# Retention into two feed-forward layers: stacked output matmuls for two pairs, small zero matmuls first, and a tile moved into pair 3

## What is computed

```python
def _attn_ref(q, k, v):
    scores = 1.0 / np.sqrt(D_) * np.matmul(q, k.transpose(0, 1, 3, 2))
    gamma = 1.0 - 2.0 ** (-5.0 - np.arange(H))
    rel = pos[:, None] - pos[None, :]
    Dmat = np.where(rel >= 0, gamma[:, None, None] ** rel[None, :, :], 0.0)
    return np.matmul(scores * Dmat[None], v)
...
for e in range(E):
    out += p[:, e:e + 1] * (np.maximum(x @ w1[e], 0.0) @ w2[e])
...
h = x @ w_in
return (h * np.tanh(log1p(exp(h)))) @ w_out
```

## Time and profile before

| what | value |
|---|---|
| median of three runs | 619.76 us |
| the profiled execution's own time | 620.43 us |
| its span (first to last instruction) | 618.7 us |
| TensorE busy | 606.0 us, 98% |
| VectorE, ScalarE, GpSimd busy | 262.9, 234.8, 278.3 us |
| matmul records | 4016 |
| granted TensorE clock, mean | 0.994 |

### The profile page before, as it was taken

One profiled execution on the slowest core, in us unless ns is written; L12 is line 12 of the kernel. 1 busy time (PEld: TensorE's weight loads), 2 busy tenths in 40 slices (PEclk: granted clock), 3 DMA queues, 4 the chain that ended last, 5 costly groups with the idle time before them and its releaser, 6 DMA issues.

```text
span 618.7 us, 9829 instructions
## 1 busy us (share of the span) xinstructions
PE 606.0 (98%) x4016; PEld 546.6 (88%) x4016; DVE 262.9 (42%) x361; ACT 234.8 (38%) x434; POOL 278.3 (45%) x230
## 2 busy tenths in 40 slices
PE   7799999999999999999999999999999999999997
PEld 4688999999899999999999999989989999989996
DVE  2468654424254424154534154535545432324334
ACT  2466333322233322223432223435455454334431
POOL 3558645534435545335553435532446543443300
PEclk9799999999999999999999999999999999999999
DMA  8963312322102332012332102321211232201002
GB/s 339 334 218 103 87 41 65 119 84 68 35 35 68 104 103 68 35 35 68 103 88 66 52 34 69 103 68 46 58 34 58 67 101 83 68 1 52 1 1 102
DMA packets 24923, 50.47 MB, mean 82 GB/s; under 512 B 2864, under 2 KB 2992, under 8 KB 24880
## 3 DMA queue, kind: packets, MB, share of 16 engines
q1 hardware_dynamic: 24736, 49.84, 25.5%
q10 hardware_dynamic: 144, 0.02, 0.0%
HBM read 47.49 MB, written 2.36 MB: 81 GB/s over the span
## 4 chain that ended last, share of the span: by engine, by line
PE 97%; issue 1%; DVE 1%; DMA 1%; ACT 0%
PE bank L494 31%; PE bank L496 31%; PE bank L495 31%; PE bank L442 2%; PE bank L470 1%; DMA loaded<-in_first 1%; PE bank L474 1%; PE bank L612 1%; PE bank L447 0%; PE bank L619 0%; DVE acc_sb L889 0%; DVE acc_sb L893 0%; ACT st L686 0%; DVE h_lo L850 0%; ACT h_hi L717 0%
## 5 line engine op out<-in xcount | busy, mean ns | idle before, releaser
L395 POOL TENSOR_TENSOR w_lo<-w_raw,w_hi 128x512 fp32r<-128x512 f32 x96 | 133.9, 1409 | 148.4 <-ACT w_hi L368 144.9
L494 PE MATMUL bank<-w_hi,h_hi 128*128 128x512 f32 x432 | 168.7, 390 | 0.0
L496 PE MATMUL bank<-w_hi,h_lo 128*128 128x512 f32 x432 | 168.4, 390 | 0.0
L495 PE MATMUL bank<-w_lo,h_hi 128*128 128x512 f32 x432 | 168.3, 390 | 0.0
L876 DVE TENSOR_TENSOR h_act<-part,bank 128x384 f32<-128x384 f32 x96 | 52.9, 551 | 170.4 <-PE bank L496 169.9
L390 POOL TENSOR_TENSOR ws<-ws_f,ws 128x1024 fp32r<-128x1024 f32 x24 | 58.4, 2432 | 144.7 <-ACT ws L364 144.7
L496 PEld LDWEIGHTS bank<-w_hi,h_lo 128*128 128x128 f32 x432 | 81.1, 188 | 16.9
L495 PEld LDWEIGHTS bank<-w_lo,h_hi 128*128 128x128 f32 x432 | 81.1, 188 | 12.3
L494 PEld LDWEIGHTS bank<-w_hi,h_hi 128*128 128x128 f32 x432 | 81.0, 188 | 12.1
L722 ACT ACTIVATE part<-bank 128x384 f32<-128x384 f32 x72 | 35.4, 491 | 138.9 <-PE bank L496 138.9
L843 DVE SCALAR_TENSOR_TENSOR h_lo<-h_act,h_hi 128x384 fp32r<-128x384 f32 x64 | 73.4, 1156 | 20.9 <-ACT h_hi L712 20.3
(11 more groups left out here) (88 smaller groups left out, 863.8 us busy)
## 6 DMA issues: line engine op xcount, KB each, us to landing
w_raw<-in_weights SPq DMA_DIRECT2D x144, 256.0 KB, 2.8
loaded<-in_toks SPq DMA_DIRECT2D x9, 512.0 KB, 6.4
loaded<-in_feats SPq DMA_DIRECT2D x8, 512.0 KB, 5.9
out<-acc_sb SPq DMA_DIRECT2D x6, 256.0 KB, 2.0
out<-acc_sb SPq DMA_DIRECT2D x1, 768.0 KB, 3.5
loaded<-in_first SPq DMA_DIRECT2D x1, 726.0 KB, 4.4
ident<-in_ident SPq DMA_DIRECT2D x1, 64.0 KB, 6.0
p_nat<-in_probs ACTq DMA_DIRECT2D x1, 18.0 KB, 6.4
```

Of the source, the lines that this page charges most:

```text
L395: pool.tensor_tensor(w_lo[layer][:, x], w_raw[:, r % RAW], w_hi[layer][:, x].bitcast(F32), ALU.subtract).then_inc(s_wl, 1)
L494: pe.matmul(out, w[0], x[0], start=first, stop=False, **more)
L495: pe.matmul(out, w[0], x[1], start=False, stop=False, **more)
L496: return pe.matmul(out, w[1], x[0], start=False, stop=last, **more)
```

## The change

In pairs 1 and 2 the state and the values of a batch are put above one another on the 128 partitions, and so are the queries and the masked scores, so that one matmul with a contraction over 128 gives what two gave. For batch 0 the state goes to the free half of the loaded values; for batch 1 it goes with the values to a new buffer `v_again`, which VectorE fills (`v_decay_again`), while GpSimd's `v_decay` handles batch 0 alone. The host lays out keys and queries of these two chunks accordingly. `masked` becomes two operations of 64 partitions for them. The seven large matmuls of zeros become 60 of 64 columns. Tile 0 moves between scores and state of pair 3 and its output, and tiles 1 to 3 each move up: behind pairs 3, 4 and 5. On VectorE `first_lo` goes ahead of `decayed` in turns 2 and 3.

```diff
+STACKED = 1, 2
-TILES_IN = {3: (0,), 4: (1,), 5: (2, 3), 6: (4,), 7: (5, 6), 8: (7,)}
+TILE_AMID = {3: 0}
+TILES_IN = {3: (1,), 4: (2,), 5: (3,), 6: (4,), 7: (5, 6), 8: (7,)}
-WARM_START, WARM_NEXT = 7, 5
+SMALL, WARM_NEXT = 60, 5
...
+        def state_and_v(c, b):
+            return v_again[:, c - 1] if b else slots[:, c % SLOTS, 2]
+        def q_and_masked(c, b):
+            return slots[:, c % SLOTS, 1 - b]
...
                 pe.wait_ge(s_vd, c + 1)
+                if c in STACKED:
+                    pe.wait_ge(s_va, c)
...
+            def of_both(c, b, h):
+                return pe.matmul(ps_o[HALF[h % 2], b, h // 2], state_and_v(c, b)[:, h], q_and_masked(c, b)[:, h],
+                                 start=True, stop=True)
...
             def output(c):
                 pe.wait_ge(s_vd, c + 1)
+                if c in STACKED:
+                    pe.wait_ge(s_xt, c)
+                    pe.wait_ge(s_st, 2 * c)
+                    pe.wait_ge(s_sm, c + 1)
+                    for hp in range(PAIRS):
+                        for b in range(BATCH):
+                            of_both(c, b, 2 * hp)
+                            mm = of_both(c, b, 2 * hp + 1)
+                    mm.then_inc(s_o, 1)
+                    return
...
+            def small_zeros(count):
+                for _ in range(count):
+                    pe.matmul(banks[7][HALF[0], 0:CH], zeros[:, 0:CH], zeros[:, 0:CH], start=True, stop=True)
...
             pe.wait_ge(s_zt, 1)
-            keep_warm(WARM_START)
+            small_zeros(SMALL)
...
                 if has_state(c):
                     scores_and_state(c)
+                if c in TILE_AMID:
+                    early_tile(TILE_AMID[c])
                 output(c)
...
                 act.wait_ge(s_kv, c + 1)
                 if c > 1:
                     act.wait_ge(s_o, c)
+                if c + 1 in STACKED:
+                    act.wait_ge(s_va, c + 1)
                 for b in range(BATCH):
-                    act.activation(st[HALF[b], c % 2], ps_state[HALF[1 - b]], ACT.Copy).then_inc(s_st, 1)
+                    to = state_and_v(c + 1, b)[HALF[1 - b]] if c + 1 in STACKED else st[HALF[b], c % 2]
+                    act.activation(to, ps_state[HALF[1 - b]], ACT.Copy).then_inc(s_st, 1)
...
+                if c in STACKED:
+                    for b in range(BATCH):
+                        op = dve.tensor_tensor(masked_scores(c, b), ps_s[c % SCORES][HALF[b]],
+                                               mask[HALF[b]].unsqueeze(1).broadcast_to([CH, HEADS, CH]), ALU.mult)
+                    op.then_inc(s_sm, 1)
+                    return
...
+            def v_decay_again(c):
+                dve.wait_ge(s_toks[c % SLOTS], landed(c))
+                by = key_decay[HALF[1], c].unsqueeze(2).broadcast_to([CH, HEADS, DH])
+                dve.tensor_tensor(v_toks(c, 1), slots[HALF[1], c % SLOTS, 2], by, ALU.mult).then_inc(s_va, 1)
...
                     for i in range(2, 5):
                         rows(i)
+                    v_decay_again(1)
+                if 1 < c <= PER_BLOCK:
+                    first_lo(c - 2)
                 if c > 0:
                     decayed(c - 1)
-                if c > 1 and c != PER_BLOCK + 1:
+                if c == 1:
+                    v_decay_again(2)
+                if c > PER_BLOCK + 1:
                     first_lo(c - 2)
```

More of the change, by code:

```diff
@@ L202, in build @@
         st = sb("st", [P, 2, HEADS, DH])
+        v_again = sb("v_again", [P, len(STACKED), HEADS, DH])
         row_decay = sb("row_decay", [P, PLACES - 1, PAIRS, CH])
@@ L247, in build @@
         s_vd = sem("s_vd")
+        s_va = sem("s_va")
         s_sc = sem("s_sc")
@@ L279, in build, with k_feats, q_feats, v_toks @@
         s_out = sem("s_out")
[L281 to L295, removed]
+        def k_feats(c, b):
+            return slots[HALF[1 - b], c % SLOTS, b] if c in STACKED else slots[HALF[b], c % SLOTS, 0]
+        def q_feats(c, b):
+            return slots[HALF[1 - b], c % SLOTS, 1 - b] if c in STACKED else slots[HALF[b], c % SLOTS, 1]
+        def v_toks(c, b):
+            return v_again[HALF[1], c - 1] if c in STACKED and b else slots[HALF[b], c % SLOTS, 2]
+        def k_toks(c, b):
+            return slots[HALF[b], c % SLOTS, 3]
+        def state_and_v(c, b):
+            return v_again[:, c - 1] if b else slots[:, c % SLOTS, 2]
+        def q_and_masked(c, b):
+            return slots[:, c % SLOTS, 1 - b]
+        def masked_scores(c, b):
+            return slots[HALF[b], c % SLOTS, 1 - b if c in STACKED else 0]
         def landed(c):
@@ L441, in score @@
             def score(c, b, h):
-                return pe.matmul(ps_s[c % SCORES][HALF[b], h], k_feats(c)[HALF[b], h], q_feats(c)[HALF[b], h],
+                return pe.matmul(ps_s[c % SCORES][HALF[b], h], k_feats(c, b)[:, h], q_feats(c, b)[:, h],
                                  start=True, stop=True)
             def state(c, b, h):
-                return pe.matmul(ps_state[HALF[1 - b], h], k_toks(c)[HALF[b], h], v_toks(c)[HALF[b], h],
+                return pe.matmul(ps_state[HALF[1 - b], h], k_toks(c, b)[:, h], v_toks(c, b)[:, h],
                                  start=c == 0 and h == 0, stop=True, skip_group_check=True)
@@ L469, in of_state @@
             def of_state(c, b, h):
-                return pe.matmul(ps_o[HALF[h % 2], b, h // 2], st[HALF[b], (c - 1) % 2, h], q_feats(c)[HALF[b], h],
+                return pe.matmul(ps_o[HALF[h % 2], b, h // 2], st[HALF[b], (c - 1) % 2, h], q_feats(c, b)[:, h],
                                  start=h < 2, stop=False, skip_group_check=True)
             def of_chunk(c, b, h):
-                return pe.matmul(ps_o[HALF[h % 2], b, h // 2], v_toks(c)[HALF[b], h], masked_scores(c)[HALF[b], h],
+                return pe.matmul(ps_o[HALF[h % 2], b, h // 2], v_toks(c, b)[:, h], masked_scores(c, b)[:, h],
                                  start=c == 0 and h < 2, stop=True, skip_group_check=True)
+            def of_both(c, b, h):
+                return pe.matmul(ps_o[HALF[h % 2], b, h // 2], state_and_v(c, b)[:, h], q_and_masked(c, b)[:, h],
+                                 start=True, stop=True)
             def output(c):
                 pe.wait_ge(s_vd, c + 1)
+                if c in STACKED:
[8 more added lines that the diff above has]
+                    return
                 if c > 0:
@@ L512, in plain_ready, with early_tile @@
                     pe.wait_ge(s_cc, ITEMS * (sums(s) - 1) + (C21, C12)[i] + 1)
+            def early_tile(t):
+                s, i = divmod(t, ITEMS)
+                plain_ready(s, i)
+                plain_products(s, i, range(KT))
             def plain_products(s, i, tiles):
@@ L631, in _ @@
                     scores_and_state(c)
+                if c in TILE_AMID:
+                    early_tile(TILE_AMID[c])
                 output(c)
                 for t in TILES_IN.get(c, ()):
-                    s, i = divmod(t, ITEMS)
-                    plain_ready(s, i)
-                    plain_products(s, i, range(KT))
+                    early_tile(t)
             for q in range(ITEMS * TT):
@@ L750, in _ @@
                         job_hi(act, job)
+                if c in TILE_AMID:
+                    plain_hi(*divmod(TILE_AMID[c], ITEMS))
                 for job in IN_TURN.get(c, ()):
@@ L812, in masked @@
                 dve.wait_ge(s_sc, c + 1)
-                dve.tensor_tensor(masked_scores(c), ps_s[c % SCORES], mask.unsqueeze(1).broadcast_to([P, HEADS, CH]),
-                                  ALU.mult).then_inc(s_sm, 1)
+                if c in STACKED:
[4 more added lines that the diff above has]
+                    return
+                dve.tensor_tensor(slots[:, c % SLOTS, 0], ps_s[c % SCORES],
+                                  mask.unsqueeze(1).broadcast_to([P, HEADS, CH]), ALU.mult).then_inc(s_sm, 1)
+            def v_decay_again(c):
+                dve.wait_ge(s_toks[c % SLOTS], landed(c))
+                by = key_decay[HALF[1], c].unsqueeze(2).broadcast_to([CH, HEADS, DH])
+                dve.tensor_tensor(v_toks(c, 1), slots[HALF[1], c % SLOTS, 2], by, ALU.mult).then_inc(s_va, 1)
             def rows(i):
@@ L950, in _ @@
                         plain_lo(*divmod(t, ITEMS))
+                if c in TILE_AMID:
+                    plain_lo(*divmod(TILE_AMID[c], ITEMS))
                 if c in ROWS_IN:
@@ L1028, in v_decay @@
                 pool.wait_ge(s_toks[c % SLOTS], landed(c))
-                pool.tensor_tensor(v_toks(c), v_toks(c), key_decay[:, c].unsqueeze(2).broadcast_to([P, HEADS, DH]),
-                                   ALU.mult).then_inc(s_vd, 1)
+                rows = HALF[0] if c in STACKED else slice(0, P)
+                v = slots[rows, c % SLOTS, 2]
+                by = key_decay[rows, c].unsqueeze(2).broadcast_to([rows.stop, HEADS, DH])
+                pool.tensor_tensor(v, v, by, ALU.mult).then_inc(s_vd, 1)
```

(5 more changed lines are left out.)

## The result

| kernel | median | lowest to highest | runs |
|---|---|---|---|
| before | 619.98 us | 619.19 to 621.02 | 20 |
| changed | 622.93 us | 618.28 to 626.23 | 20 |

The ratio is 1.0043, with an interval of 1.0029 to 1.0057: the change costs 0.4%, where 0.24% less was forecast (618.3 us, in a range of 616.6 to 621.1). It also makes the time uneven: 8 us lie between its fastest and its slowest execution, 1.8 before (up to 4.3 in the later rounds, of 23 to 35 executions). The profiled execution took 622.36 us (span 620.2), 620.43 before (618.7).

What follows compares the result with a forecast made beforehand. TensorE bounds the kernel, in the head at the pace of arriving 256-instruction code blocks. Block 7 1.7 us earlier, less 0.2 of waits, gives 1.5 us less: span 617.2, execution 618.9, median 618.3, range 616.6 to 621.1.

Steps and rivals of the forecast that it cites:

- its own signs of being wrong: Listed beforehand: zeros ending past 6.5 us, clock under 1 after 27.5, waits at other counts, steady part moved over 0.5 us.
- The bound: Only the head, the first 56 us, can change; the steady part behind it stays 562.7 us.
- the waits for code and their places: Head: TensorE waits for 256-instruction code blocks, in pair 1, at the end of scores and state 2, and in scores and state 6.
- the zeros' own time: Start of the kernel: 60 small zeros take 3.9 us, ending at 5.2 when the first load lands; cost 0.
- the stacked output's 0.94 us: Outputs of pairs 1 and 2: 32 records each taking 1.0 us, bounds 0.5 to 2.0; cost 0.
- VectorE's additions: Pairs 1 and 2: split masking and extra decays fit in VectorE's waits; uncovered, 1.3 us between scores and output.
- Rival 3: Head: waits keep number and place because data traffic, not code, causes them; no change, 619.8; chance 0.05.
- the ladder's intervals: Head, code block arrivals: block 2 at 13.0, block 3 at 18.1, 4 at 23.2, 5 at 28.9, 6 at 33.7, 7 at 40.2 us.
- the clock at tile 0: Mid pair 3: the forecast's case has tile 0 take 2.1 us from 22.7, no low clock.
- rival 2: Head: after long waits the clock stays at 1.2 GHz through tiles 0 and 1; 1.4 us slower, 621.2; chance 0.2.
- block 7's wait: Scores and state 6: TensorE ready at 37.7, block 7 at 40.2, a wait of 2.5 us giving back gain.
- The step from span to execution: Outside the span: a span of 617.2 us was taken to give an execution of 618.9 and a median of 618.3.

Runs made afterwards that it cites:

- zeros_only: The kernel before with 60 small zero matmuls in place of the seven large ones, nothing else changed: 626.66 us, ratio 1.0093.
- large_zeros_after: The changed kernel with the seven large zero matmuls back, stacked outputs and moved tiles kept: 620.90 us, ratio 1.0004 to the kernel before.
- fill_pair2: The changed kernel with ten large zero matmuls ahead of scores and state 2: 620.99 us, ratio 1.0013 to the kernel before.
- split_masked: The kernel before with masked scores of pairs 1 and 2 written by two VectorE operations of 64 partitions: 620.10 us, ratio 1.0001.
- tile4_behind5: The changed kernel with tile 4 behind pair 5 instead of pair 6: 621.46 us, ratio 1.0022 to the kernel before.
- fewer_early_loads: The changed kernel with one weight unit instead of two ahead of loads of chunks 6, 7 and 8: 621.54 us, ratio 1.0021 to before.
- tiles_back_fewer_loads: tiles_back with one weight unit instead of two ahead of chunks 6, 7 and 8: 618.94 us, ratio 0.9983 to the kernel before.
- all_three: The changed kernel with tile 4 behind pair 5, ten large zero matmuls before scores and state 2, and fewer early weight loads: 620.47 us, ratio 1.0015.
- tiles_back: The changed kernel with tiles and VectorE's order as before, stacked outputs and small zeros kept: 620.29 us, ratio 0.9989 to the kernel before.
- tile2_behind5: The changed kernel with tile 2 behind pair 5 instead of pair 4: 624.01 us, ratio 1.0055 to the kernel before.

## Why the prediction was wrong

The forecast was 618.3 us, in a range of 616.6 to 621.1, and 622.93 was measured: slower, where 1.5 us less was forecast. Two of its own signs of being wrong came true: the granted clock was under 1 after 27.5 us, and the wait in scores and state 6 ended at 43.80 us, not at 39 to 41.5.

**What held.** The bound (only the head moves, 562.4 us behind it), the waits for code and their places, the zeros' own time as free (they end at 4.66 us, ahead of the load at 5.25; their second effect, the moved boundaries, was not free, as zeros_only and large_zeros_after show), the stacked output's 0.94 us (0.117 for four records) where I took 1.0, VectorE's additions as hidden (TensorE waited 0.94 and 0.31 us for its masked scores ahead of scores and state 1 and 2, and then for code in both), and 4.3 us from block 3 to tile 0 where I had 4.6. Of the rule that crossing into a block is mostly hidden (the Trainium skill, Runtime: NRT & Kernel Launch, Instruction fetch mechanics), the runs say: so it is behind 56 us, where no profile has a wait of over 0.15 us for "issue", not in the head. Rival 3 is out, as equal counts of 256 came back in every kernel.

**The step that failed: the ladder's intervals.** "13.0 plus the mean interval of 5.1 gives 18.1" was mis-sized. Block 2 came at 13.87, since its transfer begins 4.4 us after the entering of block 1 where before it was 3.2; and as scores and state 1 began at 11.29, not 12.53, the wait for it was 1.55 us and not 0.1 to 1. The next interval was 6.1 us. A mean was the wrong choice for it: the rows of before run from 4.25 to 6.50. That the loads issued just before decide how long a block takes is likely and not shown. Of the 1.9 us by which block 3 was late, 0.9 are block 2's and 1.0 the interval's. The last interval, 6.3 us, was right (6.5). This is one profile: in those of four other kernels, the same up to block 2's transfer, block 3 came at 17.7 us, near the forecast, and in four more at 19.7 to 20.3 (the last section has both kinds). So the forecast took one of two outcomes for the only one.

**The step left out of the forecast's case: the clock at tile 0.** "From 22.7: tile 0 (2.1)" took 4.0, because the clock fell at 21.5 us, 1.5 us after the wait for block 3, and came back at 28.3. I had it as rival 2 with a chance of 0.2. Its mechanism was right, its duration less than I priced (tile 0 alone, not tile 1). Output 4 then started at 32.78 for 29.1, of which 1.6 are tile 0's start, 1.9 the clock, 0.2 the rest.

**The rest followed.** Block 6 was entered at 37.47 for 33.7, and block 7 at 43.80 for 40.2, against 41.88 before: 1.9 us later. Of these 0.4 are made good before the steady part, which leaves the 1.5 us by which the spans differ. The gain of having tile 1 done early went into block 7's wait, 1.92 us (2.5 in the forecast). The step from span to execution was mis-sized too: the forecast kept the 1.7 us between them, and with the stacked outputs it is 2.1.

The medians lie 2.9 us apart, the two profiled executions 1.9. The further microsecond goes together with executions that have more of the low clock, and fill_pair2 supports the clock as the cause; it isn't shown execution by execution, and what makes the clock fall longer in some of them stays open.

## What to carry to other kernels

Where a long unrolled program starts under heavy loads, count its instructions in 256s. Here one block came every 4.25 to 6.5 us, so it pays to put operations with much work per instruction into every block, and perhaps to issue later what is not needed yet. Removing instructions or moving a tile lost time here (2.7 and 2.3 us alone); that the cause is a boundary shifted into small work is the reading that fits. A wait that was harmless may let the clock fall over heavy work once that work is moved behind it.

## What I had not expected

- A small zero matmul came every 53 ns (60 in 3.35 us, with the last one's own 0.24 in it), below my lower bound of 57. That bound had the end of the last large one in it; they came every 427 ns, and an eighth of that is 53.
- Ten microseconds of half clock (13.3 to 23.5 us in split_masked's profile) went with a span of 616.8 us, shorter than any of 121 executions of the kernel before: no cost is seen where code was the bound.
- Kernels that are the same up to that point had the transfer of block 2 begin at 9.1 to 9.3 us in four profiles (tile4_behind5, fewer_early_loads, tiles_back_fewer_loads, all_three) and at 11.1 to 11.4 in five others, and block 3 came at 17.7 instead of 20 (in tile4_behind5, for one). Two microseconds of the head are thus open to something that was not found. It may be the chip: the three profiles of one round (tile4_behind5, tiles_back_fewer_loads, all_three) are all of the early kind and the three of another (tiles_back, fill_pair2, tile2_behind5) all of the late kind, though a third round has one of each. So the verdicts above go by ratios to the kernel before of the same round, not by single profiles.
